# Unit 0's leaf chain on VectorE ahead of the joined weights, expert weights split during round 0, unit 1 loaded padded, and a new table of places

## The reference

```python
def _attn_ref(q, k, v, f_logit):            # (4, 8, 768, 48) each
    f = 1.0 / (1.0 + np.exp(-f_logit))
    state = np.zeros((B, H, D, D), dtype=np.float32)
    for t in range(S):
        state = f[:, :, t, :, None] * state + np.einsum('bhd,bhe->bhde', k[:, :, t], v[:, :, t])
        y[:, :, t] = np.einsum('bhd,bhde->bhe', q[:, :, t], state)
    return y.astype(np.float32)

def _moe_ref(x, w_in, w_out):               # w_in 384 x 2048, w_out 2048 x 384
    h = x @ w_in
    g = np.where(h >= 1, h, np.where(h <= -1, 0.0, (h + 1) ** 2 / 4))
    return (g @ w_out).astype(np.float32)

def _moe2_ref(x, w1, w2, w3, w_out):        # w1, w2 384 x 1024, w3 1024 x 1024, w_out 1024 x 384
    a = x @ w1
    b = x @ w2
    h = a * b @ w3
    return (h @ w_out).astype(np.float32)
```

## Time and profile before

| what | value |
|---|---|
| median of 3 executions | 978.04 us (977.85 to 978.16) |
| the profiled execution, its own time | 978.19 us |
| its span, first to last instruction | 976.5 us |
| TensorE busy | 910.6 us, 93% |
| VectorE, ScalarE, GpSimd busy | 582.0, 421.4, 176.3 us |
| mean granted TensorE clock | 0.967 |

### The profile page before, as it was taken

One profiled execution on the slowest core, in us unless ns is written; L12 is line 12 of the kernel. 1 busy time (PEld: TensorE's weight loads), 2 busy tenths in 40 slices (PEclk: granted clock), 3 DMA queues, 4 the chain that ended last, 5 costly groups with the idle time before them and its releaser, 6 DMA issues. The chain is left out here.

```text
span 976.5 us, 21801 instructions
## 1 busy us (share of the span) xinstructions
PE 910.6 (93%) x9288; PEld 873.6 (89%) x9288; DVE 582.0 (60%) x1128; ACT 421.4 (43%) x853; POOL 176.3 (18%) x179
## 2 busy tenths in 40 slices
PE   2982389999999999999999999999999999999998
PEld 2972389999999999999999999998999999999997
DVE  3568978878888887887888874463222222222221
ACT  3233254474474464564654644573222232222221
POOL 6506721412503403403313100000000000000000
PEclk9995579999999999999999999999999999999999
DMA  9537041060060150240330100501011011010000
GB/s 287 181 108 203 1 83 41 3 135 14 13 136 2 27 122 2 51 98 2 77 71 3 50 2 3 232 11 74 1 49 49 1 49 49 1 50 25 1 25 25
DMA packets 105425, 57.51 MB, mean 59 GB/s; under 512 B 83056, under 2 KB 100976, under 8 KB 104816
## 3 DMA queue, kind: packets, MB, share of 16 engines
q1 hardware_dynamic: 105328, 56.11, 21.1%
HBM read 45.09 MB, written 11.01 MB: 57 GB/s over the span
## 5 line engine op out<-in xcount | busy, mean ns | idle before, releaser
L1270 DVE TENSOR_TENSOR product<-bank,a_copy 128x384 f32<-128x384 f32 x64 | 35.7, 557 | 226.2 <-PE bank L1296 226.2
L1086 PE MATMUL bank<-x_hi,w_in_hi 128*128 128x384 f32 x384 | 136.9, 356 | 0.2 <-DVE x_lo L912 0.2
L1086 PE MATMUL bank<-g_hi,w_out_hi 128*128 128x384 f32 x384 | 133.4, 347 | 0.0
L1294 PE MATMUL bank<-y_hi,w_hi 128*128 128x384 f32 x384 | 129.9, 338 | 2.3 <-SPq L1212 2.3
L1296 PE MATMUL bank<-y_hi,w_lo 128*128 128x384 f32 x384 | 129.7, 338 | 0.0
L1295 PE MATMUL bank<-y_lo,w_hi 128*128 128x384 f32 x384 | 129.6, 337 | 0.0
L1088 PE MATMUL bank<-x_hi,w_in_lo 128*128 128x384 f32 x384 | 129.3, 337 | 0.0
L1087 PE MATMUL bank<-x_lo,w_in_hi 128*128 128x384 f32 x384 | 129.2, 337 | 0.0
L1088 PE MATMUL bank<-g_hi,w_out_lo 128*128 128x384 f32 x384 | 129.0, 336 | 0.0
L1087 PE MATMUL bank<-g_lo,w_out_hi 128*128 128x384 f32 x384 | 128.5, 335 | 0.0
L643 ACT ACTIVATE g_hi<-gated 128x384 fp32r<-128x384 f32 x128 | 67.2, 525 | 126.6 <-DVE gated L918 126.6
(11 more groups left out here) (121 smaller groups left out, 1826.6 us busy)
## 6 DMA issues: line engine op xcount, KB each, us to landing
v_leaf<-in_v_dram SPq DMA_DIRECT2D x8, 576.0 KB, 5.5
v_rows<-in_v_dram SPq DMA_DIRECT2D x64, 72.0 KB, 2.7
middle<-middle_out SPq DMA_DIRECT2D x8, 576.0 KB, 2.8
out_dram<-out_rows SPq DMA_DIRECT2D x8, 576.0 KB, 3.3
w_rows<-in_moe_w_dram SPq DMA_DIRECT2D x8, 512.0 KB, 7.7
f_leaf<-in_f_logit_dram SPq DMA_DIRECT2D x24, 144.0 KB, 3.1
k_leaf<-in_k_dram SPq DMA_DIRECT2D x24, 144.0 KB, 3.4
q_leaf<-in_q_dram SPq DMA_DIRECT2D x24, 144.0 KB, 3.4
```

The costliest lines, as they stand in the source:

```text
L1086: nc.tensor.matmul(o, w[0], b[0], start=first, stop=False)
L1270: nc.vector.tensor_tensor(pf[:, f % RING], b_bank[f % 2][:, 0:UNIT], af[:, f % 2], ALU.mult)\
L1294: nc.tensor.matmul(o, w[0], b[0], start=first, stop=False)
```

## The change

**Placement of unit 0.** `STAGED` goes from 2 to 1: only unit 0 goes through `raw`. Its score0, prefix and query4 move from GpSimd to VectorE (score0 and query4 as one instruction of 96x1536 each), and its copy of k to ScalarE. The chain stands ahead of the split of the last weights and of the first turned rows on VectorE. Its score lags get a buffer of their own, `first_score_lags`. The clearing of `scores` (1536 columns) goes to VectorE's start.

**Unit 1** is loaded by `load_ahead`, as later units are. Its DMAs stand on SyncE's queue behind w3's block 4 and ahead of blocks 5 to 7.

**Expert weights.** All 14 pieces are VectorE's (`GPSIMD_PIECES = ()`). Their order is three w_in pieces (first half of the columns), three w_out pieces, three w_in pieces, five w_out pieces, and TensorE waits for each piece where it first needs it. w_out comes by four DMAs instead of two, behind the last joined row. Nine pieces have places in round 0.

**Places.** The joins and the leaf chain of unit 1 get new places, and so do some steps of every round.

The core of the diff:

```diff
-STAGED = 2
+STAGED = 1
+GPSIMD_PIECES = ()
...
-        maskf = place("masks_float", [P, 2, 2, W], over="scores")
+        maskf = place("masks_float", [P, 2, 2, W], over="k_rows")
...
+        sl_first = place("first_score_lags", [PT, VCOLS, H, D], over="w_in_hi")
...
-                  for kk in range(KD) for c in range(0, F1, F1 // 2)]
...
+                  for c in range(0, F1, F1 // 2) for kk in range(KD)]
+        WO_LOADS = 4
+        halves_in = pieces
+        pairs_out = [(tuple(w[:, t:t + 2, :].rearrange(flat) for w in (*wo, wo_raw)), KD + WO_LOADS * t // T1)
+                     for t in range(0, T1, 2)]
+        pieces = halves_in[0:KD] + pairs_out[0:KD] + halves_in[KD:] + pairs_out[KD:]
...
-        STAGE_AT = ((5, 6, 8), (11, 13, 14))
-        LEAF_AT, KROW_AT, UPDATE_AT, Y_AT, X_AT = (5, 8, 13), (17, 21), (19, 25), (22, 23, 28), (23, 28, 29)
+        STAGE_AT = ((5, 6, 7), (11, 13, 15))
+        LEAF_AT, KROW_AT, UPDATE_AT, Y_AT, X_AT = (5, 6, 15), (17, 18), (19, 25), (22, 23, 28), (23, 28, 29)
...
             def load_w3(t):
...
+            load_first()
+            sp.dma_start(wl_raw[:], w_last.rearrange("(t p) n -> p t n", p=P)).then_inc(w_last_in, 16)
+            for t in range(4):
+                load_w3(t)
+            load_values(0, 0)
             load_rows(0, 0, 0)
             for kk in range(KD):
                 sp.dma_start(wi_raw[:, kk], w_in[kk * P:(kk + 1) * P, :]).then_inc(w_landed[kk], 16)
+            load_w3(4)
+            load_ahead(0, 1, 1)
+            for t in range(5, T2):
+                load_w3(t)
...
+            sp.wait_ge(joined_out, 16 * T2)
+            for n in range(WO_LOADS):
...
                 if n == 0:
-                    wait(act, "gates", 1, 1)
-                    wait(act, "k_in", 1, 16 * LEAF)
-                    wait(act, "q_in", 1, 16 * LEAF)
-                    act.wait_ge(joined_out, 16 * T2)
+                    wait(act, "leaf_add", 0, 3)
...
+                elif kind == "score0" and u < STAGED:
+                    wait(dve, "q_in", u, 16 * LEAF)
+                    wait(dve, "k_in", u, 16 * LEAF)
+                    nc.vector.tensor_tensor(yl[:], qj, kj, ALU.mult).then_inc(sems["score0"], 4)
+                elif kind == "prefix" and u < STAGED:
+                    wait(dve, "gates", u, 1)
+                    wait(dve, "carry", u, 3)
+                    for j in range(1, LEAF):
+                        if j > 1:
+                            wait(dve, "prefix", u, j - 1)
+                        nc.vector.tensor_tensor(fj[:, j], fj[:, j], fj[:, j - 1], ALU.mult).then_inc(sems["prefix"], 1)
+                elif kind == "query4" and u < STAGED:
+                    wait(dve, "score_lag", u, 3)
+                    wait(dve, "prefix", u, 3)
+                    nc.vector.tensor_tensor(qj, qj, fj, ALU.mult).then_inc(sems["query4"], 4)
...
+                if u == 0 and i % (T1 // 2) == 0:
+                    for n in range(KD):
+                        wait_low(pe, in_piece(2 * i // T1, n))
...
+                if u == 0 and i % 2 == 0:
+                    wait_low(pe, out_piece(i))
```

More of the change, by code:

```diff
@@ L342, in tokens_in @@
             eng.wait_ge(raw_in[n], 16 * (u + 1))
-            if later(u):
-                wait(eng, "k_tr" if name == "k_in" else "q_tr", u - 1, PAIRS)
             copy(dst, first_tokens(n)).then_inc(sems[name], 16 * LEAF)
@@ L366, in low_weights, with wait_low @@
             eng.wait_ge(w_hi, n + 1)
-            on.tensor_tensor(lo, raw, hi.bitcast(F32), ALU.subtract).then_inc(w_lo[n % 2], 1)
+            on.tensor_tensor(lo, raw, hi.bitcast(F32), ALU.subtract).then_inc(w_lo[n not in GPSIMD_PIECES], 1)
+        def wait_low(eng, n):
+            on_vector = n not in GPSIMD_PIECES
+            eng.wait_ge(w_lo[on_vector], sum((m not in GPSIMD_PIECES) == on_vector for m in range(n + 1)))
         block = ctx.enter_context(nc.Block())
@@ L411, in store, with load_first @@
                 sp.sem_inc(middle_free, 1)
-            def load_first(half):
+            def load_first():
                 for n, t in enumerate((f_logit, k, q)):
-                    if half:
-                        wait(sp, ("gates", "k_in", "q_in")[n], 0, (1, 16 * LEAF, 16 * LEAF)[n])
-                    src = rows(t, 0, half).rearrange("h (p j) d -> p h (j d)", j=LEAF)
+                    src = rows(t, 0, 0).rearrange("h (p j) d -> p h (j d)", j=LEAF)
                     if n:
@@ L422, in load_first, with load_w3 @@
                         sp.sem_inc(sems["f_in"], 16 * (LEAF - 1))
-            load_first(0)
-            sp.dma_start(wl_raw[:], w_last.rearrange("(t p) n -> p t n", p=P)).then_inc(w_last_in, 16)
-            for t in range(T2):
+            def load_w3(t):
                 if t >= 4:
@@ L493, in ahead @@
                 kind = step[0]
-                if kind == "score0":
-                    if u < STAGED:
-                        tokens_in(pool, nc.gpsimd.tensor_copy, kj, 1, "k_in", u)
+                if kind == "score0" and u >= STAGED:
                     wait(pool, "q_in", u, 16 * LEAF)
                     wait(pool, "k_in", u, 16 * LEAF)
-                    if later(u):
-                        wait(pool, "leaf_tr", u - 1, KD)
+                    wait(pool, "leaf_tr", u - 1, KD)
                     for j in range(LEAF):
@@ L503, in ahead @@
                             .then_inc(sems["score0"], 1)
-                elif kind == "prefix":
+                elif kind == "prefix" and u >= STAGED:
                     wait(pool, "carry", u, 3)
@@ L510, in ahead @@
                             .then_inc(sems["prefix"], 1)
-                elif kind == "query4":
+                elif kind == "query4" and u >= STAGED:
                     wait(pool, "score0", u, 4)
@@ L551, in main @@
                         wait(act, "tot_ev", u, 1)
-                        wait(act, "leaf_add", u, 3)
                         if later(u):
+                            wait(act, "leaf_add", u, 3)
                             wait(act, "q_next", u - 1, 2)
@@ L614, in ahead @@
                     wait(act, "f_in", u, 16 * LEAF)
-                    if 0 < u < STAGED:
-                        wait(act, "tot_tr", u - 1, 1)
-                        wait(act, "query4", u - 1, 4)
                     nc.scalar.activation(fj, first_tokens(0) if u < STAGED else fj, ACT.Sigmoid)\
                         .then_inc(sems["gates"], 1)
+                elif step[0] == "first_q" and u < STAGED:
+                    tokens_in(act, lambda to, src: nc.scalar.activation(to, src, ACT.Copy), kj, 1, "k_in", u)
             def split_x(u):
@@ L809, in main @@
                         wait(dve, "q_ev", u, PAIRS)
-                        wait(dve, "leaf_add", u, 3)
+                        if later(u):
+                            wait(dve, "leaf_add", u, 3)
                     else:
@@ L944, in weights @@
                 for n in pieces_at(pos):
-                    if n % 2:
+                    if n not in GPSIMD_PIECES:
                         low_weights(dve, nc.vector, n)
@@ L1137, in turn_of_units @@
             def turn_of_units(u):
-                if u == 0:
-                    for done in w_lo:
-                        pe.wait_ge(done, WI_PIECES // 2)
                 if u < UNITS:
@@ L1147, in turn_of_units @@
                     up(1, u)
-                if u == 0:
-                    for done in w_lo:
-                        pe.wait_ge(done, len(pieces) // 2)
             pe.wait_ge(constants, CONSTANTS)
```

72 lines of the change are left out of this document (36 added, 36 removed).

## The result

The changed kernel takes **964.63 us** (median of 4, 963.41 to 965.12), the kernel before 978.10 beside it (977.85 to 978.65): a ratio of 0.986 [0.9843, 0.9877]. The forecast was 960.5, range 951 to 971. The profiled execution took 964.89 us, with a span of 963.2.

What follows compares the result with a forecast made beforehand. TensorE was taken to bound the rounds; in the prologue it waits for VectorE at a slow clock. 978.19 - 20.7 (prologue) + 3.0 + 0.3 (round 0) = 960.8 profiled, 960.5 as median; range 951 to 971, forecast case 955 to 966 at 0.55.

Steps and rivals of the forecast that it cites:

- (1): Prologue up to the first join: turn 1 at 27.7 us, join 0 at 29.3, including 2.0 lost meeting GpSimd's `values`.
- (2): Prologue up to the first masked copy: leaf_lag parts end at 38.5 us, masks last at 46.4, copy done at 48.6.
- (3): Prologue up to krow 0: at 74.1 us, with 2.5 for meeting GpSimd's score0 and 1.5 for a slower clock.
- (4): Prologue up to y 0: 22.4 us to 96.5; krow 1's 11.9 us wait gone because it stands before the update.
- (5): Prologue from y 0 to the experts: last x sum 13 us later at 109.5 (bounds 12 to 16.2), round 0 at 111.1.
- w_out's landing: End of the prologue: w_out's first quarter, some 9 us, thinly covered; if it took 12.1, x_hi comes 4 us later.
- Round 0: First round: nine new weight pieces make TensorE late by 3.0 us (bounds 0 and 7), moved transposition of f adds 0.3.
- Rounds 1 to 7: Later rounds: moved steps use VectorE's idle time, 11.8 us free a round, and cost 0.
- rival C: Every round stalls at `up` or `down`; 3 us in seven rounds cancels the gain, 3.5 gives 985; chance 0.04.
- A: Less lost: GpSimd meetings cost 2.9 us instead of 5.8, clock stays 2.4 GHz, round 0 absorbs its pieces; 952.1, chance 0.20.
- B: More lost in the prologue: clock falls twice or more and w_out's landing holds up x_hi; 971, chance 0.13.
- D: Prologue: the wait only moves from attention to the joins; only 8.5 us and some 3 go; 970, chance 0.06.

Runs made afterwards that it cites:

- experiment 1: Changed kernel with the masks made at GpSimd's start instead of behind the leaf values: 961.93 us.
- experiment 7: Changed kernel with krow 1 back behind update 0, as before the change: 961.78 us.
- experiment 8: Kernel before the change, with krow 1 moved ahead of update 0 and nothing else: 978.35 us.
- experiment 6: Changed kernel with joins 2 to 7 and their turns back, one after another, ahead of unit 0's first score matmuls: 980.02 us.
- experiment 3: Changed kernel with w_in pieces three to six meant to stand beside joins 6 and 7, and the last five w_out pieces spread over round 0: 971.27 us.
- experiment 4: Changed kernel with the six weight pieces of positions 7 to 12 of round 0 made by GpSimd instead of VectorE: 963.69 us.
- experiment 5: Changed kernel with the low halves of round 0's nine weight pieces not computed, ScalarE writing plain copies instead: 965.30 us.
- experiment 10: Changed kernel with masks at GpSimd's start, krow 1 behind update 0, w_in pieces three to six behind turn 7, last five w_out pieces spread over round 0: 961.99 us.
- experiment 9: Kernel before the change, with GpSimd's three w_in pieces given to VectorE: 976.99 us.
- experiment 2: Changed kernel with the last weights' low half and join 0 ahead of the second lag step: 964.62 us.
- experiment 12: Changed kernel with early masks, late krow 1, joins one place earlier but joins 6 and 7 behind y 0 and y 1, two w_out pieces later: 954.88 us.
- experiment 11: Changed kernel with masks at GpSimd's start, krow 1 behind update 0, and every join one place earlier: 956.18 us.

## Why the prediction was right, and where it was off

The time lies inside the range and inside the forecast's own 955 to 966. The forecast's 20.7 us of gain came out as 19.8.

- **(1) To the first join.** Turn 1 at 27.15 (27.7), join 0 at 28.74 (29.3). `values` of unit 0 started at 23.27, not 20.9, since v landed late, and the meeting cost VectorE 1.2 us (4.82 against 3.60), not 2.0. GpSimd paid as well: 4.62 against 3.20.
- **(2) To the first masked copy.** Both leaf_lag parts ended at 38.6 (38.5). The masks were last, as said, and 2.3 us later (48.67 against 46.4), because the select loop took 9.64 us. The 7.39 of the earlier trace rows was no price of the loop: it is 5.14 when VectorE is idle (experiment 1).
- **(3) krow 0** at 73.69 (74.1). The 2.3 us were regained: the meeting of `k_cols` with score0 of unit 1 cost 0.8 (2.17 against 1.36), not 2.5, which is 1.7 of them; the rest is spread over the other terms, and that the sum comes out so close is in part luck.
- **(4) y 0** at 96.59 (96.5), joins 4 to 7 back to back. The reason I gave for the vanished 11.9 us was wrong. That the wait is gone because krow 1 stands before the update falls with experiments 7 and 8: by itself the place moves the wait to y 0 (9.61 us there), and in the changed kernel the other place is better. With the joins dense again, and krow 1 early as in experiment 8, TensorE waits 2.68 us for the state (experiment 6): some 7 of the 9.6 us went with what else differs between these two kernels. The rows point to VectorE's order, which now reaches the state behind two lag instructions instead of six, three pieces and two reductions; no run has that order alone. The joins cover what is left.
- **(5)** The last x sum ended at 110.31 (109.5), 13.7 us behind y 0 (13, bounds 12 to 16.2), and the first expert matmul stood at 112.03 (111.1). w_out's landing was hidden.
- **Round 0** is the term that was mis-sized: +5.02 us where I had 3.0 and 0.3. TensorE is idle for 4.04 us (68.92 busy of 72.96): 0.40 ahead of the first expert matmul, then 0.33, 0.42, 0.34, 0.88, 0.34 and 0.18 from 125 to 154 us, and 1.15 at 168.8 for y_rows (I had 0.5, 0.2, 1.0 and 1.2). I had followed VectorE's queue alone. Experiment 7 puts the 1.15 down to the place of krow 1. That the others come from the pieces' crowding is read from the order and not shown: experiments 3, 4, 5 and 10, which moved the pieces, each made new waits of their own. The other 0.98 is more busy time (68.92 against 67.94), of which some 0.3 is the transposition of f; the rest stays open.
- **Rounds 1 to 7** cost nothing, as said: rival C did not occur.
- **The second part** has 1.56 us that no step foresaw (below). 0.9 + 1.7 + 1.5 us are the 4.1 between 960.8 and the profiled 964.89.

**The rivals.** A was right in part: two of the three meetings were cheaper on VectorE than I took them (1.2 and 0.8 for 2.0 and 2.5; the leaf_lag parts ended as priced), but the clock fell and round 0 did not absorb its pieces. B's clock falls came (47 to 56 us, and 103 to 114), without w_out's landing. C's sum was off: by the forecast of 960.5 the gain is 17.5 us and would be gone at 2.5 us a round, not 3. D took the 8.5 us row as a gain that would stay in any case; experiment 9 gives it 1.95 us at most by itself.

**What the gain hangs on.** Single parts are worth little: without the spread joins all the others together bring the start 3.7 us forward, which round 0's 5.3 us take back (experiment 6), and in the old order of joins the long instruction and the place of krow 1 give 1.95 and 0.7 us of the start and no change of the median that is clear of noise (experiments 9 and 8). A part of the chain that is shortened hands its time to the next wait, unless TensorE has other work there. With the joins beside attention TensorE is busy for 37.3 of the 44 us from 57 to 101, at a granted clock of 1.00; before and behind that stretch it still falls (0.50 over 47 to 56 and over 103 to 114 us).

## What to carry to other kernels

When one engine alternates with another and waits, look first for work that can stand in all the waits at once; shortening single waits along such a chain mostly lengthened the next one here. Look also at what the other engine has queued ahead of the result that is waited for. Price the clock with it: work taken out of the gaps cost its own time here, and the lower clock of what stayed behind (1.56 us for 0.89). Before a place is filled on one engine, follow every engine of that loop through it (here ScalarE's ramp and VectorE's gate), and take the price of an instruction from a row in which nothing met it.

## What the runs showed of the hardware that I had not expected

- **A waiting engine can be kept out over several instructions of the other, and it can be let in between two.** `k_cols` on VectorE took 9.88 us from 86.30, while GpSimd ran seven instructions without a pause from 84.17 to 94.97; none of the four products among them was longer than 1.00 us. In experiment 9 the same instruction met the same four products at the same place (86.35, products from 84.22) and took 2.02, and one of the products took 2.13 instead of 1.00: here it was let in. It also goes the other way. In experiment 9 VectorE ran lag steps and six weight pieces without a pause, and the first of GpSimd's three prefix products beside them took 8.2 us, the other two 1.0 each; in the changed kernel, where VectorE idled, the three took 3.22 together. The Trainium skill, SBUF — State Buffer, in "SBUF: two separate sides", says that whichever of the two starts first has the shared port pair for the whole instruction. The rows agree that it is no even split. They do not show what decides who has the pair next, so a meeting with a stream has no single price: `k_cols`, 1.35 us alone, took 2.02, 2.17, 3.00 and 9.88.
- **GpSimd's select loop** of 24 instructions took 5.14 us with VectorE nearly idle (experiment 1), 7.39 and 9.64 with VectorE at work. Which VectorE instructions stretch it was not tried.
- **The same 2.3 us wait ends at either clock.** At the start of the second part TensorE waits 2.29 to 2.31 us in the profiled execution of every kernel. In the changed kernel and in experiments 1, 2, 5 and 12 the clock then falls (0.63 to 0.69 over the first 4 us), and the part takes 1.5 us longer; in the kernel before and in the other eight it is 1.00:

```profile
644.00:648.00 4.00, 4.00 (x23) 4.00 (x24) 0.46 (x1) 0.49 (x1) 0.00 (x0) 1.00 0.59 221
```

  (This one is experiment 11.) The same instructions stand ahead of it in all. The start times show no order (644.00, 649.55, 651.63 and 660.85 keep the clock, 642.99, 649.82, 652.55 and 654.69 lose it), so why is open. With one profile of each kernel it is open too whether the kernel or the single execution decides; 1.5 us of a comparison of two profiled executions can be this.
